# Hash step of the next head moved two tiles earlier on TensorE, with ScalarE and VectorE reordered to match

## The reference

```
q_bits = (q @ proj > 0); k_bits = (k @ proj > 0)          # 6 bits each
mask   = bucket(q_bits)[:, None] == bucket(k_bits)[None, :]
scores = where(mask, q @ k.T / 8, -1e9)
attn   = exp(scores - max(scores)); attn /= attn.sum() + 1e-9
out    = attn @ v
```

## Time and profile before

| | |
|---|---|
| median of 3 runs | 804.47 us |
| profiled execution | 804.34 us, span 802.6 us |
| mean granted TensorE clock | 0.977 |
| TensorE (PE) busy | 755.7 us, 94% |
| VectorE (DVE) busy | 439.8 us, 55% |
| ScalarE (ACT) busy | 357.3 us, 45% |
| GpSimd (POOL) busy | 233.1 us, 29% |
| chain of waits that ended last | PE 85%, ACT 4%, POOL 3%, DMA 3%, issue 2%, DVE 2% |

### The profile page before, as it was taken

One profiled execution on the slowest core, in us unless ns is written; L12 is line 12 of the kernel. 1 busy time (PEld: TensorE's weight loads), 2 busy tenths in 40 slices (PEclk: granted clock), 3 DMA queues, 4 the chain that ended last, 5 costly groups with the idle time before them and its releaser, 6 DMA issues.

```text
span 802.6 us, 11427 instructions
## 1 busy us (share of the span) xinstructions
PE 755.7 (94%) x4141; PEld 622.3 (78%) x4141; DVE 439.8 (55%) x703; ACT 357.3 (45%) x543; POOL 233.1 (29%) x225
## 2 busy tenths in 40 slices
PE   3899999999999995799999999859999999999998
PEld 2677777777777764799999999748888888888886
DVE  4677777877787788456665555533443223222222
ACT  1454556666555553255665555432332323232223
POOL 3158676576767671321211111100000000000000
PEclk9899999999999998699999999979999999999999
DMA  5674444544544302756666765180010100010001
GB/s 124 186 201 100 108 97 116 116 110 103 119 104 104 87 11 56 252 178 221 197 203 224 258 225 190 57 314 5 0 53 1 52 1 1 1 52 1 1 0 53
DMA packets 70163, 85.97 MB, mean 107 GB/s; under 512 B 42223, under 2 KB 44271, under 8 KB 69616
## 3 DMA queue, kind: packets, MB, share of 16 engines
q1 hardware_dynamic: 64784, 74.99, 32.5%
q0 software_dynamic: 2560, 7.34, 2.8%
q10 hardware_dynamic: 2784, 3.18, 1.1%
HBM read 58.76 MB, written 13.63 MB: 90 GB/s over the span
## 4 chain that ended last, share of the span: by engine, by line
PE 85%; ACT 4%; POOL 3%; DMA 3%; issue 2%; DVE 2%; SPq 0%; POOLq 0%; ACTq 0%; DVEq 0%
PE score_ps L1439 11%; PE score_ps L1441 11%; PE score_ps L1440 11%; PE out_pair L1441 7%; PE out_pair L1439 7%; PE out_pair L1440 7%; PE out_pair L1307 4%; PE score_ps L1254 4%; PE out_pair L1309 3%; PE out_pair L1308 3%; ACT probs L727 3%; PE score_ps L1283 3%; PE out_pair L1331 3%; POOL probs_lo L629 2%; PE score_ps L1291 2%
## 5 line engine op out<-in xcount | busy, mean ns | idle before, releaser
L629 POOL TENSOR_TENSOR probs_lo<-probs,probs_hi 128x768 fp32r<-128x768 f32 x60 | 109.1, 1856 | 89.4 <-ACT probs_hi L731 89.4
L1439 PE MATMUL score_ps<-w_hi,h_hi 128*128 128x512 f32 x320 | 126.1, 394 | 0.4 <-DVE h_lo L1203 0.4
L1441 PE MATMUL score_ps<-w_hi,h_lo 128*128 128x512 f32 x320 | 124.7, 390 | 0.0
L1440 PE MATMUL score_ps<-w_lo,h_hi 128*128 128x512 f32 x320 | 124.6, 389 | 0.0
L1196 DVE SCALAR_TENSOR_TENSOR gated<-tclip,out_pair 128x512 f32<-128x512 f32 x48 | 33.1, 689 | 145.2 <-ACT tclip L858 145.2
L1439 PE MATMUL out_pair<-xT_hi,w_hi 128*128 128x512 f32 (+1 forms) x320 | 112.1, 350 | 0.0
L1441 PE MATMUL out_pair<-xT_hi,w_lo 128*128 128x512 f32 (+1 forms) x320 | 110.9, 347 | 0.0
L1440 PE MATMUL out_pair<-xT_lo,w_hi 128*128 128x512 f32 (+1 forms) x320 | 110.9, 347 | 0.0
L858 ACT ACTIVATE tclip<-out_pair,three 128x512 f32<-128x512 f32 x48 | 33.1, 690 | 146.5 <-PE out_pair L1441 146.5
L934 DVE TENSOR_REDUCE rowmax<-score_ps 128x1 f32<-128x768 f32 x96 | 88.7, 952 | 15.8 <-PE score_ps L1254 15.4
L1141 DVE TENSOR_TENSOR w_lo<-w_raw,w_hi 128x1024 fp32r<-128x1024 f32 x72 | 85.9, 1222 | 18.4 <-ACT w_hi L741 18.0
(11 more groups left out here) (182 smaller groups left out, 1302.1 us busy)
## 6 DMA issues: line engine op xcount, KB each, us to landing
w_raw<-in_moe_w SPq DMA_DIRECT2D x32, 1024.0 KB, 9.3
w_raw<-in_moe_w_in SPq DMA_DIRECT2D x4, 1024.0 KB, 7.9
w_raw<-in_moe_w_out SPq DMA_DIRECT2D x4, 1024.0 KB, 12.5
qk_raw<-in_q SPq DMA_DIRECT2D x16, 192.0 KB, 3.8
qk_raw<-in_k SPq DMA_DIRECT2D x16, 192.0 KB, 3.9
v_raw<-in_v SPq DMA_DIRECT2D x16, 192.0 KB, 2.5
k_ext<-q_ext SPq DMA_DIRECT2D x16, 192.0 KB, 2.6
k_pair<-q_ext SPq DMA_DIRECT2D x16, 192.0 KB, 3.1
```

Source lines behind the costliest of these rows:

```text
L629: g.tensor_tensor(probs_lo[:, kc, :], probs[:, kc, :], probs_hi[:, kc, :].bitcast(F32), ALU.subtract).then_inc(lo_done_p, 1)
L1439: mm(out_tile, lhs[0], rhs[0], start=first, stop=False)
L1440: mm(out_tile, lhs[0], rhs[1], start=False, stop=False)
L1441: return mm(out_tile, lhs[1], rhs[0], start=False, stop=last)
```

## The change

Three orders are changed; no instruction is added or removed.

- TensorE: hash_qk moves from behind values(2) to between max_tile 2 and max_tile 3.
- ScalarE: high_qk moves from behind high_probs of tile 3 to behind high_probs of tile 2.
- VectorE: bits moves from behind take_max 4 to in front of it.

```
@@ ScalarE, head()
                 for kc in range(BY_V, C):
                     if not first:
                         high_probs(h.prev(), kc)
-                    if kc == BY_V + 1 and not last:
+                    if kc == BY_V and not last:
                         high_qk(h.next())
@@ VectorE, head()
                 take_max(h, 2)
                 take_max(h, 3)
-                take_max(h, 4)
                 if not last:
                     bits(h.next())
+                take_max(h, 4)
                 take_max(h, 5)
                 minus_max(h)
@@ TensorE, head()
                 values(1)
                 max_tile(h, 2, first)
+                prepare(hash_qk)
                 max_tile(h, 3, first)
                 values(2)
-                prepare(hash_qk)
                 max_tile(h, 4, first)
```

## The result

The changed kernel takes 814.86 us, against 804.50 for the kernel before: ratio 1.0130, 95% interval 1.0106 to 1.0152. The forecast was 814.5, range 810.5 to 818. Its profiled execution took 815.20 us with a span of 813.4. In the later sessions (chips 0 and 8) the kernel before measured 2 to 3 us more (medians 806.6 to 807.5). The changed one, measured there once more beside it, did not: 814.3, ratio 1.0081, interval 1.0066 to 1.0096. The two intervals do not meet, so the size of the difference, unlike its sign, depends on the session. The experiments say where that can come from.

A forecast was written before the change was run, and what follows sets the result against it. TensorE was taken to bound the heads, busy 254.97 of 256 us. Ten heads at 0.65, four at 0.72 and 0.7 for head 0 gave 10.1 us on 804.34, so 814.5 us; range 810.5 to 818.

The forecast's parts named there:

- the stall at the hash: TensorE, heads 1 to 14: hash_qk reached at 145.90 must wait for qk_lo until 146.56; 0.72 us stall per head.
- ScalarE, gain nothing: ScalarE's high_qk, moved up by one, still waits for the transposes and starts at 144.71 either way; gain nothing.
- GpSimd 0.70 to 0.77 later: GpSimd's stream follows the later high_probs of tile 3: 0.77 us later per head, about 0.70 on the other side.
- values(5) was just in time: TensorE starts values(5) at 151.18, just after GpSimd's low parts end at 151.08; GpSimd's delay adds at most 0.05 us.
- the two delays lie on top of each other: At values(5), GpSimd's lateness (151.95) and TensorE's hash stall (151.90) overlap, so at most 0.05 us is added.
- minus_max held by the blend: VectorE's L939 and L940 wait for GpSimd's later blend; turn_max starts 0.69 us later, so middle heads pay about that.
- VectorE, gain nothing: Bits and the DMA behind them come 0.7 us earlier on VectorE, but nobody was waiting for them; gain nothing.
- The sum: Whole kernel: ten middle heads at 0.65, four heads at 0.72 and head 0 at 0.7 make 10.1 us more.
- Head 0: First head: two row maxima behind bits cost 0.90 us at turn_max, 0.45 may return through the clock; taken as 0.7.
- minus_max misses its gap: Rival: L942 is also held for GpSimd's x_rows; ten middle heads pay a further 1.1 us each, about 825; chance 0.07.

The follow-up runs named there:

- hash_one_tile: Kernel before with hash_qk moved only half the way, between max_tile 3 and values(2); ScalarE and VectorE unchanged: 812.29 us, ratio 1.0072.
- after_turn_first: The changed kernel with turn_qk put before values(0) on TensorE instead of behind it: 810.97 us, ratio 1.0053 against the kernel before.
- scalar_only: Kernel before with only ScalarE's move, high_qk one place earlier: 814.97 us, ratio 1.0098.
- tensor_vector: Kernel before with TensorE's and VectorE's moves, hash_qk and bits, ScalarE unchanged: 815.95 us, ratio 1.0117.
- vector_only: Kernel before with only VectorE's move, bits in front of take_max 4: 808.63 us, ratio 1.0024.
- tensor_only: Kernel before with only TensorE's move, hash_qk behind max_tile 2: 818.39 us, ratio 1.0143.
- tensor_scalar: Kernel before with TensorE's and ScalarE's moves, bits left behind take_max 4: 817.77 us, ratio 1.0140.
- before_again: The kernel before, unchanged, measured and profiled again in a later session: 807.55 us, ratio 1.0003.
- after_again: The changed kernel, unchanged, measured again beside the kernel before on the same chip: 814.30 us, ratio 1.0081.
- run 14: Not a label of a kernel: in "both run 14 matmuls" the word run is a verb, and 14 counts matmuls from 30 to 34 us.

## Why the prediction was right

**TensorE, the stall at the hash.** Forecast: the hash 2.71 us behind the start of the transposes (143.85 to 146.56), 0.66 us of standing and 0.06 for the first matmul. Measured 2.71 (148.99 to 151.70), 0.67, and 0.05 (0.28 instead of 0.23 us to the next matmul). hash_one_tile and after_turn_first give the cause by two separate ways.

**ScalarE, gain nothing; GpSimd 0.70 to 0.77 later.** Measured: q_ext starts 0.85 us behind the transposes' start, 0.86 before; GpSimd's second low part comes 2.51 us behind its first instead of 1.82: 0.69. That values(5) was just in time, and that the two delays lie on top of each other, was the least certain step. scalar_only shows the first and tensor_vector the second.

**minus_max held by the blend.** Forecast 0.69 later at turn_max, turn_mean to turn_back near 1.6. Measured 10.05 us behind the transposes' start against 9.43 (0.62 later, as GpSimd is 0.69 later and not 0.77), and 1.63. L939 let go at the end of v_lo and L940 at that of the blend, as in head 2 before. TensorE's own wait there was forecast as 0.16 us (153.81 to 153.97) and is 0.06 (0.87 behind turn_mean instead of 0.81): the 0.37 + 0.35 of the forecast is 0.09 short of the 0.81 that TensorE takes from turn_mean to turn_max when nothing holds it.

**VectorE, gain nothing.** vector_only agrees for the middle heads, and bits starts 5.36 us behind the transposes' start (154.35), 5.37 by the forecast. The step did not see what the move does where GpSimd is in time: with TensorE's move alone minus_max is held a second time, by x_rows, in eight heads (tensor_only), and with VectorE's move as well it is not, but for head 2 (tensor_vector). In the change ScalarE's move already sees to that (tensor_scalar). The rival "minus_max misses its gap" was put on the wrong kernel; it is real in TensorE's move alone and in head 2 of several kernels, in one profile also of the kernel before.

**The sum.** Forecast 0.65 in ten heads and 0.72 in four. In the first two profiles heads 2 to 14 take 8.12 us more (46.90 to 278.35 before, 49.15 to 288.72 after), where the forecast's terms for these thirteen make 8.7. The ten heads 3 to 12 take 6.48 more, 0.65 each, as said; heads 2, 13 and 14 take 0.38, 0.69 and 0.57, where 0.72 was said. So the term of the middle heads is right to 0.01, and that of heads 2, 13 and 14 up to 0.34 too high.

Head 0 was forecast as 0.9 at turn_max, of which half was to come back through the clock. The 0.9 is right: 0.86 in the two profiles that start at the low level (before_again and after_again), and 0.81 in the two that start at the high one (27.14 before, 27.95 in tensor_vector, whose head 0 has the program of the change). What comes back depends on when the clock rises, which the forecast had to assume. Up to turn_back of head 1 the change costs 2.00 us in the first of these pairs, where the rise comes 2.1 us later, and 0.97 in the second (46.90 and 47.87), where it comes at 34.5 and 34.2 us. The forecast's terms for heads 0 and 1, 0.7 and 0.72, make 1.42, between two cases neither of which is near it. In the pair of first profiles it is 2.25 (46.90 and 49.15), because the changed kernel started at the low level and the kernel before did not: the first two matmuls of the hash start 0.49 and 0.29 us apart.

So the whole fits in part by luck. In the first two profiles 2.25 up to turn_back of head 1, 8.12 in heads 2 to 14 and 0.5 behind the heads (490.0 and 490.5 us from the last turn_back to the end of the span) make 10.9, where the forecast had 1.4, 8.7 and nothing. The 0.5 lies within what two profiles of the kernel before differ by there (490.0 and 491.0). Where the kernel before is at 807.5, the same 814.3 is 6.8 us more and not 10.1: the predicted time stands, the predicted difference is that of an execution without the loss in heads 2 and 3.

The Trainium skill, page "TensorE: Matmul & The Clock Gate", section "Architectural detail", says that TensorE's queue can pull weight loads ahead of running matmuls. The trace shows no help from it at this wait: in the kernel after, the weight loads of L1240 themselves wait 11.5 us for VectorE's qk_lo, in the same 14 places.

## What to carry to other kernels

A step may be moved up only as far as its inputs allow: add up the chain of its producers from their own first wait (here transposes, q_ext and qk_lo, 2.71 us) and set it against the work that lies between (here 2.04 us up to the end of max_tile 2); what is missing is the stall. Moving the producers' place in other queues doesn't shorten a chain in which each link already starts within 0.05 us of the end of the one before. And a step in a queue with idle time isn't free: ask for the one behind it that is just in time, since a 0.7 us delay on GpSimd was worth nearly 8 us by itself, and nothing once another stall of that size covered it.

## What was not expected of the hardware

- The smallest VectorE operations on SBUF ([128, 6], 0.17 us) are held until the running GpSimd operation is over: 0.77, 0.95 and 1.06 us, ending 0.03 us behind it, in L939, L940 and L942 alike. In the fourteen profiles 316 of these operations are longer than 0.25 us, and each ends 0.02 to 0.04 us behind the end of a GpSimd operation; of the 356 shorter ones none starts with more than 0.25 us of a GpSimd operation left. The row maxima from PSUM (0.96 us) and qk_lo (0.96 us) keep their length beside GpSimd.
- The granted clock reads 1.00 from 20 to 24 us in the profiles of before, before_again and after_again, yet in the last two the hash's matmuls at 21.4 us start 0.48 and 0.43 us apart, in the first 0.29 and 0.23. From 30 to 34 us it reads 0.50 in before and 1.00 in before_again, and both run 14 matmuls in these 4 us. Up to its first change the column doesn't show the level that the execution starts in; the distance of matmul starts does.
- A wait of 0.87 us at turn_max of head 2 was followed by a stretch at the lower clock in before_again, which cost 2.7 us, three times the wait, and by a shorter one in hash_one_tile. In vector_only and tensor_scalar the same 0.87 us left the clock at 1.00, and head 3 took 17.8 and 18.5 us. What decides between the two isn't shown. The stalls of 0.67 us in every head of the changed kernel never brought the clock down.
